# Masks added by TensorE for the first five attention units, in a fused attention and mixture-of-experts kernel

## The chip, the cores and the metric

The kernel runs on one core of a Trainium2 chip. The metric is the device time of one execution in microseconds, median of several runs. An engine is named by what it does here: TensorE multiplies (matmul and transpose) into PSUM, VectorE (DVE) and ScalarE (ACT) read PSUM and SBUF, GpSimd (POOL) works on SBUF alone, SyncE (SP) issues most DMAs.

## The reference, cut to what matters

Three layers, one after the other: masked attention, a dense layer pair, and a sparse expert layer with skipping. The change touches only the attention of batch 0.

```python
# q, k, v: (4, 8, 576, 64)
rel = pos[:, None] - pos[None, :]
mask_local   = (rel >= 0) & (rel < 32)                         # heads 0..3
mask_strided = (rel >= 0) & (pos[None] % 32 == pos[:, None] % 32)  # heads 4..7
scores = where(mask, q @ k.T / sqrt(64), -1e9)
attn = exp(scores - max(scores)); attn /= sum(attn) + 1e-9
x = attn @ v                                       # 2304 x 512
h = x @ w_in                                       # 512 -> 2048
g = where(h >= 1, h, where(h <= -1, 0, (h + 1)**2 / 4))
x = g @ w_out                                      # 2048 -> 512
# then: rows with x @ w_skip <= 0 stay; the others go through one of 8 experts
```

## The kernel before, in words

**Units.** Attention is cut into units: one batch, one pair of heads (a "pair", one head in each half of the 128 partitions), and a few query tiles. Pairs 0 and 1 are local: a tile is 96 queries by 128 keys, so a unit of four tiles has scores of 96 x 512 for each head of the pair. Pairs 2 and 3 are strided: queries and keys are sorted by position modulo 32 on the host, a tile is 72 x 72, a unit is 72 x 288 for each head. Units 0 and 1 are local, 2 to 5 strided; all six belong to batch 0 and stand ahead of the main loop. The two heads are called halves below (`hh` 0 and 1).

**Jobs.** Each engine has a written order of jobs for the six units ahead of the loop (the strings `PE_BEFORE`, `DVE_BEFORE`, `ACT_BEFORE`, `POOL_BEFORE`), executed strictly in that order. The letters:

- S, TensorE (L845): score products of a unit, 16 matmuls in 64-row tiles, into two banks of PSUM.
- M, VectorE (L1177, L1181): for each half one scalar_tensor_tensor reads the bank, multiplies by 1/8, adds the mask and writes `prob_first` in SBUF; then for each half a negated maximum of every row of every tile, into `row_max`. The bank is free after the first of these.
- D, GpSimd (L1735): for unit 5 only, adds the negated maximum to the scores.
- X, ScalarE (L1577): exponentials in `prob_first`, one instruction for each tile, with the negated maximum as bias; for unit 5 (L1572) one for each half.
- K, GpSimd (L1745, L1748): partial sums of the rows of units 0 and 1. E, VectorE: the sums and their reciprocals.
- G, GpSimd (L1755): scales the exponentials by the reciprocals.
- P, TensorE (L861): transposes; C, ScalarE (L1590): copies them out of the bank. V, TensorE (L881): times the values. H, ScalarE (L1598) and L, VectorE (L1219): the result x as a rounded part and a rest.
- W, ScalarE (L1637) and R, GpSimd (L1785): the first `w_in` tiles as a rounded part and a rest.

**Banks.** PSUM has eight banks; `bank_table()` gives them to S (two), P (two) and V (one) jobs in rotation. A job waits until the use before it on its bank has been read out (`take_bank`).

**Fillers.** `FILLERS` says how many products of 128x512 bfloat16 on the tile `warm` (L825) stand ahead of a job. They compute nothing; "Q" is the second half of a P job. The list starts after eight more such products.

**Loop.** 96 steps follow (six chunks of 384 tokens, 16 feature tiles each): TensorE does `hidden` (L1042, twelve products) and `output` (L1058) and between them the jobs of later attention units, at places of `places_of_chunk`. The first step needs the results of all six units (`x_hi_ready`, `x_ready`) and the first weight remainder R0. Unit 6 and 7 are the rest of the local pairs of batch 0. Unit 8 (S at place 7 of chunk 0, after step 3's first half) is the first of batch 1 and waits for its own load of q and k, which SyncE issues after all weights.

**Loads.** SyncE issues loads in one written order (the first q and k, the identity, more q and k with the strided mask between them, v, three tiles of `w_in`, one of `w_out`, the rest of q, k, v, then the remaining weights alternately, then batch 1). ScalarE issues two: the first keys, and the local mask (L1681). VectorE waits for the local mask before its first job.

The code that the diff touches:

## Time and profile before

| | us |
|---|---|
| median of 3 runs | 503.79 (503.68 to 503.83) |
| the profiled execution | 503.48 |
| its span | 501.7 |
| TensorE busy | 493.4 (98%) |
| TensorE weight loads | 426.3 (85%) |
| VectorE busy | 251.8 (50%) |
| ScalarE busy | 192.9 (38%) |
| GpSimd busy | 218.1 (43%) |

The span is the stretch between the first and the last instruction of the profiled execution; the execution's own time is 1.8 us longer. Busy shares are means over the whole span. The stage ahead of the loop lasts about 26.6 us and has quite other shares than the rest, so it has to be read by windows. Instructions of one engine overlap a little at their ends, so that the distance from start to start is shorter than the duration that the rows show. The ends of matmuls are modelled. "issue" in a chain is time in which the engine waited for nothing that the profile shows, and "DVEq" is the instruction queue of VectorE.

### The profile page before, as it was taken

The page shows a single profiled execution, that of the slowest core. Times are in us where ns is not written, and L with a number is a line of the kernel's source. Part 1 is how long each engine was busy: PE and PEld are TensorE (multiplying, and loading weights), DVE is VectorE, ACT ScalarE, POOL GpSimd, SP SyncE. Part 2 cuts the span into 40 slices and gives each one's busy share as a digit, 9 for nine tenths or more (in the row PEclk, how much of TensorE's full clock was granted, in tenths as well). Part 3 has the DMA queues.
Part 4 walks back from the last instruction along what each step waited for, and adds up shares of the span by engine and source line. Part 5 has one row for each costly group of instructions (what it writes and reads, how often), then busy time and mean ns, then how long its engine had stood idle before and what let it go on. Part 6 is the DMA issues. An engine that isn't in the chain of part 4 may idle for free.

```text
span 501.7 us, 8901 instructions
## 1 busy us (share of the span) xinstructions
PE 493.4 (98%) x3429; PEld 426.3 (85%) x3429; DVE 251.8 (50%) x593; ACT 192.9 (38%) x429; POOL 218.1 (43%) x245
## 2 busy tenths in 40 slices
PE   8999999999999999999999999999999999999996
PEld 4688888889988888888888888888998898888895
DVE  5876657634335536666525666652445342332322
ACT  4956456543223324353423343442322222222222
POOL 2978966852223324465423555642222312222221
PEclk9999999999999999999999999999999999999999
DMA  8993220103001204202110421000300017850001
GB/s 282 354 386 110 73 78 5 52 2 127 0 7 42 74 25 174 80 2 82 49 48 15 160 82 33 1 2 18 125 2 1 1 40 297 294 169 1 2 0 67
DMA packets 18977, 42.15 MB, mean 84 GB/s; under 512 B 2054, under 2 KB 3920, under 8 KB 18932
## 3 DMA queue, kind: packets, MB, share of 16 engines
q1 hardware_dynamic: 18580, 41.13, 23.9%
q8 instruction: 28, 0.46, 0.4%
q10 hardware_dynamic: 256, 0.41, 0.3%
q14 instruction: 17, 0.14, 0.1%
q0 software_dynamic: 96, 0.02, 0.0%
HBM read 32.94 MB, written 8.78 MB: 83 GB/s over the span
## 4 chain that ended last, share of the span: by engine, by line
PE 93%; DVE 3%; ACT 2%; POOL 1%; issue 1%; DVEq 0%
PE bank L1058 39%; PE bank L1042 39%; PE bank L881 4%; PE bank L845 4%; PE bank L861 3%; PE bank L825 1%; PE bank L985 1%; PE bank L966 1%; POOL part_sums L1745 1%; DVE prob L1193 1%; ACT g_hi L1704 0%; DVE bank L1186 0%; DVE row_max L1191 0%; POOL part_sums L1748 0%; ACT prob L1580 0%
## 5 line engine op out<-in xcount | busy, mean ns | idle before, releaser
L1824 POOL TENSOR_TENSOR g_lo<-act_f,g_hi 128x384 fp32r<-128x384 f32 x96 | 97.3, 1014 | 197.1 <-ACT g_hi L1704 196.6
L1695 ACT ACTIVATE act_f<-act_f,half_col 128x384 f32<-128x384 f32 x96 | 59.1, 615 | 201.0 <-DVE act_f L1431 200.9
L1431 DVE TENSOR_SCALAR act_f<-bank 128x384 f32<-128x384 f32 x96 | 53.3, 555 | 146.5 <-PE bank L1042 141.5
L1042 PE MATMUL bank<-x_hi,win_hi 128*128 128x384 f32 x384 | 87.7, 347 | 0.6 <-DVE act_f L1434 0.6
L1058 PE MATMUL bank<-wout_hi,g_hi 128*128 128x512 f32 x285 | 85.0, 406 | 0.0
L1704 ACT CAST g_hi<-act_f 128x384 fp32r<-128x384 f32 x96 | 49.1, 512 | 92.0 <-DVE act_f L1434 91.7
L1042 PE MATMUL bank<-x_hi,win_lo 128*128 128x384 f32 x384 | 83.9, 337 | 0.0
L1042 PE MATMUL bank<-x_lo,win_hi 128*128 128x384 f32 x384 | 83.2, 335 | 0.0
L1058 PE MATMUL bank<-wout_lo,g_hi 128*128 128x512 f32 x285 | 81.1, 393 | 0.0
L1058 PE MATMUL bank<-wout_hi,g_lo 128*128 128x512 f32 x285 | 81.0, 392 | 0.0
L1042 PEld LDWEIGHTS bank<-x_hi,win_hi 128*128 128x128 f32 x384 | 66.7, 188 | 8.3 <-issue 1.5
L1434 DVE TENSOR_TENSOR act_f<-act_f,bank 128x384 f32<-128x384 f32 x96 | 52.5, 547 | 36.7 <-ACT act_f L1695 33.1
L1042 PEld LDWEIGHTS bank<-x_hi,win_lo 128*128 128x128 f32 x384 | 69.6, 188 | 0.0
L1042 PEld LDWEIGHTS bank<-x_lo,win_hi 128*128 128x128 f32 x384 | 68.1, 188 | 0.2 <-DVEq L1222 0.2
L1058 PEld LDWEIGHTS bank<-wout_lo,g_hi 128*128 128x128 f32 x285 | 53.5, 188 | 12.6
L1058 PEld LDWEIGHTS bank<-wout_hi,g_lo 128*128 128x128 f32 x285 | 53.5, 188 | 12.3
L1058 PEld LDWEIGHTS bank<-wout_hi,g_hi 128*128 128x128 f32 x285 | 49.9, 188 | 6.8 <-issue 0.6
L1755 POOL TENSOR_TENSOR prob<-prob,row_sum 72x288 f32<-72x288 f32 (+2 forms) x52 | 37.8, 746 | 23.5 <-DVE row_sum L1214 23.5
L1735 POOL TENSOR_TENSOR prob<-prob,row_max 72x288 f32<-72x288 f32 (+1 forms) x32 | 25.7, 821 | 28.0 <-DVE row_max L1181 28.0
L1219 DVE TENSOR_TENSOR x_lo<-bank,x_hi 128x288 fp32r<-128x288 f32 (+2 forms) x32 | 18.8, 586 | 30.3 <-ACT x_hi L1598 29.7
L1208 DVE TENSOR_REDUCE sum_terms<-prob 72x4 f32<-72x288 f32 (+2 forms) x52 | 23.2, 487 | 5.0 <-ACT prob L1580 5.0
L1790 POOL TENSOR_TENSOR wout_lo<-wout_raw,wout_hi 128x512 fp32r<-128x512 f32 x16 | 20.5, 1284 | 10.8 <-ACT wout_hi L1641 10.8
(135 smaller groups left out, 423.4 us busy)
## 6 DMA issues: line engine op xcount, KB each, us to landing
w_early<-in_w_dram SPq DMA_DIRECT2D x4, 2048.0 KB, 9.0
qk<-in_qk_dram SPq DMA_DIRECT2D x12, 592.0 KB, 4.9
out_dram<-y_rows SPq DMA_DIRECT2D x18, 256.0 KB, 2.6
win_raw<-in_w_in_dram SPq DMA_DIRECT2D x16, 256.0 KB, 9.3
wout_raw<-in_w_out_dram SPq DMA_DIRECT2D x16, 256.0 KB, 9.6
y_dram<-y_rows SPq DMA_DIRECT2D x15, 256.0 KB, 3.0
v<-in_v_dram SPq DMA_DIRECT2D x6, 384.0 KB
v<-in_v_dram SPq DMA_DIRECT2D x6, 288.0 KB
```

The source lines that it names most:

```text
L845: mm = pe.matmul(bank_of("S", n, hh)[0:rows, width * i:width * (i + 1)], buf[head, q_at:q_at + rows], buf[head, k_at:k_at + width], start= ...
L1042: mm = pe.matmul(h_ps[s % 2][:, 0:CH], w[:, f, P * k:P * (k + 1)], x[:, k, cols], start=(at == 0), stop=(at == len(order) - 1))
L1058: mm = pe.matmul(y_ps[t][:, :], g[:, s % RING, P * t:P * (t + 1)], w[:, f, :], start=(f == 0 and i == 0), stop=(f == FT - 1 and i == 2))
L1208: dve.tensor_reduce(sum_terms[0:unit_rows(u), hh, 0:u.nt, 0], tiled(u, hh), AX.X, ALU.add)\
L1431: dve.tensor_scalar(tile, h_ps[s % 2][:, 0:CH], -1.0, 1.0, ALU.max, ALU.min).then_inc(clip_ready, 1)
L1434: dve.tensor_tensor(tile, tile, h_ps[s % 2][:, 0:CH], ALU.max).then_inc(act_ready, 1)
L1695: act.activation(tile, tile, ACT.Square, bias=half_col[:, 0:1], scale=0.5).then_inc(square_ready, 1)
L1704: act.copy(g_hi[:, s % RING, :], tile).then_inc(g_hi_ready, 1)
L1735: pool.tensor_tensor(tiled(u, hh), tiled(u, hh), over_tiles(u, peak_of(u, hh)), ALU.add)\
L1755: pool.tensor_tensor(tiled(u, hh), tiled(u, hh), over_tiles(u, sums_of(u, hh)), ALU.mult)\
L1790: pool.tensor_tensor(wout_lo[:, f, :], wout_raw[:, f, :], wout_hi[:, f, :].bitcast(F32), ALU.subtract)\
L1824: pool.tensor_tensor(g_lo[:, s % RING, :], act_f[:, s % 2, :], g_hi[:, s % RING, :].bitcast(F32), ALU.subtract).then_inc(g_lo_ready, 1)
```

## The change

For units 0 to 4 (`PE_MASKS = 5`) the mask is no longer added by VectorE:

- TensorE's S job ends with one more product for each half: the identity (in bfloat16) times the mask tile (in bfloat16, 0 or -2^33), accumulated onto the scores in the bank. 2^33 is large enough that the later factor 1/8 leaves it below -1e9.
- VectorE's M job becomes, for each half, a negated maximum straight from the bank (96x512 or 72x288), a wait for it, and a multiplication of these maxima by 1/8 (96x4 or 72x4).
- ScalarE's X job reads the bank instead of `prob_first`, with scale 1/8 and the scaled maximum as bias, and writes `prob_first`. The bank is free only when the exponentials of its half are done: the semaphore `exp_ready` stands in for `bank_free`.
- Three constants are added to the constant table (local mask, identity, strided mask as bfloat16 pairs in float32 words). ScalarE's second DMA loads them as one tile `mask_words` of 96 x 448 words in place of the float32 local mask (96 x 512 words). SyncE loads the float32 local mask later, after the first `w_out` tile (unit 6 waits for it), and the float32 strided mask after the q and k of pairs 2 and 3.
- The four orders and the fillers are new. Fillers ahead of the loop, beyond the first eight: 34 before, 30 after. V0 stands before P1, P3 before V1, V3 before P5; VectorE has E3 before M5 and L0 before E5; ScalarE swaps W0 and H0, and C4 and H3; GpSimd has G3 before D5.

```diff
--- before.py
+++ after.py
@@ -36,6 +36,7 @@
 TILES_UP = -(-SLOTS // SPAN) * SPAN
 FAR = float(1 << 17)
 MASKED = -1e9
+FAR_BELOW = -float(1 << 33)
 SCRATCH = 4096
 
 CH = 384
@@ -88,6 +89,7 @@
 UNITS = all_units()
 N_PRO = 6
 SHIFTED = 5
+PE_MASKS = 5
 POOL_SUMS = 2
 REST = 2
 PER_BATCH = 8
@@ -112,13 +114,13 @@
 
 
 
-PE_BEFORE = "S0 S1 S2 S3 S4 P0 S5 P1 V0 P2 V1 P3 V2 V3 P4 P5 V4 V5"
-DVE_BEFORE = "M0 M1 M2 E0 M3 E1 M4 E2 M5 E3 E4 E5 L0 L1 L2 L3 L4 L5"
-ACT_BEFORE = "X0 X1 X2 X3 C0 X4 W0 C1 C2 H0 X5 C3 H1 H2 H3 C4 C5 H4 H5 W1 W2"
-POOL_BEFORE = "K0 K1 G0 G1 G2 D5 G3 G4 G5 R0 R1 R2"
-
-
-FILLERS = {("S", 1): 2, ("S", 2): 6, ("P", 0): 14, ("Q", 0): 2, ("P", 1): 2, ("Q", 1): 1, ("P", 2): 1, ("V", 1): 2, ("P", 3): 1, ("P", 5): 1, ("V", 4): 2}
+PE_BEFORE = "S0 S1 S2 S3 S4 P0 S5 V0 P1 P2 P3 V1 V2 P4 V3 P5 V4 V5"
+DVE_BEFORE = "M0 M1 M2 E0 M3 E1 M4 E2 E3 M5 E4 L0 E5 L1 L2 L3 L4 L5"
+ACT_BEFORE = "X0 X1 X2 X3 C0 X4 H0 C1 C2 W0 X5 C3 H1 H2 C4 H3 C5 H4 H5 W1 W2"
+POOL_BEFORE = "K0 K1 G0 G1 G2 G3 D5 G4 G5 R0 R1 R2"
+
+
+FILLERS = {("S", 1): 2, ("S", 2): 6, ("P", 0): 12, ("Q", 0): 2, ("V", 0): 1, ("P", 1): 1, ("Q", 1): 2, ("P", 2): 1, ("V", 1): 1, ("P", 5): 1, ("V", 4): 1}
 
 
 def jobs_of(names):
@@ -213,6 +215,13 @@
 
 BANKS, PRO_USES = bank_table()
 
+READ_BY_EXP = {BANKS["S", n][hh]: (n, hh) for n in range(PE_MASKS) for hh in range(2)}
+
+
+def frees(bank, use):
+
+    return use - sum(b == bank and k <= use for b, k in READ_BY_EXP)
+
 
 def constants():
     r = np.arange(P)
@@ -223,11 +232,17 @@
     strided_mask = (res[:, None] == res[None, :]) & (pos[:, None] >= pos[None, :])
     fill = lambda keep: np.where(keep, 0.0, MASKED)
     token = r[:, None] + P * np.arange(NT)[None, :]
+    as_bf16 = lambda a: (np.ascontiguousarray(a, dtype=np.float32).view(np.uint32) >> 16).astype(np.uint16)
+    in_words = lambda a: as_bf16(a).view(np.float32)
+    far = lambda keep: np.where(keep, 0.0, FAR_BELOW)
     parts = {
         "ident": np.eye(P),
         "mask_local": np.concatenate([fill(first)] + [fill(local)] * 3, axis=1),
         "mask_strided": np.concatenate([fill(strided_mask)] * 4, axis=1),
         "add_groups": (r[:, None] % GROUP == np.arange(E + 1)[None, :]) * 1.0,
+        "local_words": in_words(np.concatenate([far(first)] + [far(local)] * 3, axis=1)),
+        "ident_words": in_words(np.eye(TQ)),
+        "strided_words": in_words(np.concatenate([far(strided_mask)] * 4, axis=1)),
         "from_here": (r[:, None] >= r[None, :]) * 1.0,
         "ones": np.ones((P, P)),
         "expert_order": np.tile(np.arange(E, 0, -1)[None, :], (P, 1)),
@@ -330,6 +345,18 @@
         assert at <= steps_end
         prob_t_first = [sb(f"prob_t_first{i}", [P, 2, 4 * TQ], F32, offset=prob_at + 4 * 2 * 4 * TQ * i)
                         for i in range(2)]
+
+
+        words_from = columns["local_words"][0]
+        words = {n: (columns[n][0] - words_from, columns[n][1], columns[n][2])
+                 for n in ("local_words", "ident_words", "strided_words")}
+        n_words = sum(width for _, _, width in words.values())
+        assert n_words <= S
+        mask_words = sb("mask_words", [TQ, n_words], F32, offset=x_at + 4 * S)
+
+        def in_bf16(name):
+            at, rows, width = words[name]
+            return mask_words[0:rows, at:at + width].bitcast(BF16)
 
         mask_l = sb("mask_l", [TQ, 4 * TK], F32)
         mask_s = sb("mask_s", [TS, 4 * TS], F32)
...
@@ -536,17 +564,21 @@
 
         def wait_free(eng, kind, n, i=0):
             bank, use = BANKS[kind, n][i]
-            eng.wait_ge(bank_free[bank], use)
+            eng.wait_ge(bank_free[bank], frees(bank, use))
 
         def take_bank(eng, kind, n, i=0):
             bank, use = BANKS[kind, n][i]
-            if use > 1:
-                eng.wait_ge(bank_free[bank], use - 1)
+            if (bank, use - 1) in READ_BY_EXP:
+                unit, hh = READ_BY_EXP[bank, use - 1]
+                eng.wait_ge(exp_ready, 2 * unit + hh + 1)
+            elif use > 1:
+                eng.wait_ge(bank_free[bank], frees(bank, use - 1))
 
         def wait_pro_banks(eng, which):
             for bank in which:
                 if PRO_USES[bank] > 0:
-                    eng.wait_ge(bank_free[bank], PRO_USES[bank])
+                    assert (bank, PRO_USES[bank]) not in READ_BY_EXP
+                    eng.wait_ge(bank_free[bank], frees(bank, PRO_USES[bank]))
 
 
         def qk_of(u):
@@ -692,9 +724,9 @@
             sp.dma_start(qk_main[0][:, 0:4 * TQ], qk[0, 0, :, 0:4 * TQ]).then_inc(qk_loaded[0], 16)
             constant(ident, "ident", ident_loaded)
             first_tiles(1)
-            constant(mask_s, "mask_strided", mask_s_loaded)
             load_qk(0, 2)
             load_qk(0, 3)
+            constant(mask_s, "mask_strided", mask_s_loaded)
             for p in range(2):
                 sp.dma_start(v_main[p][:, 0:4 * P], v[0, p, :, 0:4 * P]).then_inc(v_loaded[p], 16)
             load_v(0, 2)
@@ -702,6 +734,7 @@
             for f in range(3):
                 load_w_in(f)
             load_w_out(0)
+            constant(mask_l, "mask_local", mask_l_loaded)
             rest_tiles(0)
             rest_tiles(1)
             sp.dma_start(w_score[:, :, :], w_score_dram[:, :, :]).then_inc(scores_loaded, 16)
@@ -844,9 +877,16 @@
                         head = slice(D * hh, D * hh + D)
                         mm = pe.matmul(bank_of("S", n, hh)[0:rows, width * i:width * (i + 1)],
                                        buf[head, q_at:q_at + rows], buf[head, k_at:k_at + width],
-                                       start=True, stop=True)
-                        if i == u.nt - 1:
+                                       start=i == 0 or n >= PE_MASKS, stop=n >= PE_MASKS)
+                        if i == u.nt - 1 and n >= PE_MASKS:
                             mm.then_inc(full_sem("S", n, hh), 1)
+                if n < PE_MASKS:
+                    if n == 0:
+                        pe.wait_ge(mask_words_loaded, 16)
+                    for hh in range(2):
+                        pe.matmul(bank_of("S", n, hh)[0:rows, 0:u.nt * width], in_bf16("ident_words")[0:rows, 0:rows],
+                                  in_bf16("strided_words" if strided(u.p) else "local_words"), start=False,
+                                  stop=True).then_inc(full_sem("S", n, hh), 1)
 
             def transpose_probs(n):
                 u = UNITS[n]
@@ -1161,10 +1201,21 @@
             def masked_scores(n):
                 u = UNITS[n]
                 cols = u.nt * unit_width(u)
+                if n < PE_MASKS:
+                    for hh in range(2):
+                        wait_full(dve, "S", n, hh)
+                        by_tile = scores_of(u, hh).rearrange("p (i w) -> p i w", w=unit_width(u))
+                        dve.tensor_reduce(peak_of(u, hh), by_tile, AX.X, ALU.max, negate=True).then_inc(peaks_ready, 1)
+                        dve.wait_ge(peaks_ready, 2 * n + hh + 1)
+                        dve.tensor_scalar(peak_of(u, hh), peak_of(u, hh), D ** -0.5, None, ALU.mult)\
+                           .then_inc(max_ready, 1)
+                    return
                 if strided(u.p):
                     dve.wait_ge(mask_s_loaded, 16)
                     mask = mask_s[:, :]
                 else:
+                    if n == N_PRO:
+                        dve.wait_ge(mask_l_loaded, 16)
                     mask = mask_l[:, 0:cols] if u.t0 == 0 else mask_l[:, TK:TK + cols]
                 if N_PRO <= n < N_PRO + 2:
                     wait_full(dve, "V", n - N_PRO)
@@ -1415,7 +1466,6 @@
             dve.memset(half_col[:, :], 0.5).then_inc(half_ready, 1)
             dve.memset(sum_terms[:, :, :, :], 1e-9).then_inc(terms_ready, 1)
             dve.wait_ge(terms_ready, 1)
-            dve.wait_ge(mask_l_loaded, 16)
             for kind, n in jobs_of(DVE_BEFORE):
                 if kind == "M":
                     masked_scores(n)
@@ -1572,9 +1622,11 @@
                         a = act.activation(prob_of(u, hh), prob_of(u, hh), ACT.Exp)
                     elif n < SHIFTED:
                         act.wait_ge(max_ready, 2 * n + hh + 1)
+                        width = unit_width(u)
                         for i in range(u.nt):
-                            tile = tiled(u, hh)[:, i, :]
-                            a = act.activation(tile, tile, ACT.Exp, bias=peak_of(u, hh)[:, i:i + 1])
+                            scored = bank_of("S", n, hh)[0:unit_rows(u), width * i:width * (i + 1)]
+                            a = act.activation(tiled(u, hh)[:, i, :], scored, ACT.Exp,
+                                               bias=peak_of(u, hh)[:, i:i + 1], scale=D ** -0.5)
                     else:
                         act.wait_ge(shift_ready, 2 * (n - N_PRO) + hh + 1)
                         a = act.activation(prob_of(u, hh), prob_of(u, hh), ACT.Exp)
@@ -1677,8 +1729,8 @@
 
             act.dma_start(qk_main[0][:, QC:QC + PAD + 4 * TQ], qk[0, 0, :, QC:QC + PAD + 4 * TQ])\
                .then_inc(qk_loaded[0], 16)
-            at, rows, width = columns["mask_local"]
-            act.dma_start(mask_l[:, :], table_dram[0:rows, at:at + width]).then_inc(mask_l_loaded, 16)
+            act.dma_start(mask_words[:, :], table_dram[0:TQ, words_from:words_from + n_words])\
+               .then_inc(mask_words_loaded, 16)
             for kind, n in jobs_of(ACT_BEFORE):
                 if kind == "X":
                     exponentials(n)
```

## Rows read from the trace of the kernel before

**Rows 1.** The page, part 4: the chain that ended last, by engine.

```profile
PE 93%; DVE 3%; ACT 2%; POOL 1%; issue 1%; DVEq 0%
```

**Rows 2.** Busy microseconds in two stretches: engines PE, PEld, DVE, ACT, POOL, clock, DMA.

```profile
10.00:15.00 5.00, 4.03 (x42) 2.05 (x39) 4.86 (x17) 5.00 (x20) 4.76 (x9) 1.00 1.03 292
26.50:43.00 16.50, 15.93 (x106) 13.56 (x104) 12.19 (x30) 11.36 (x26) 13.81 (x14) 1.00 0.87 325
```

**Rows 3.** The chain in order of time, 0 to 30 us: start, duration, what.

```profile
5.78 1.28 DVE prob_first L1177 x2
...
7.70 1.29 ACT prob_first L1577 x4
...
13.95 1.01 POOL prob_first L1755
...
16.55 0.67 PE bank L845 x16
...
18.64 0.81 PE bank L881 x16
...
26.61 2.41 PE bank L1042 x12
```

**Rows 4.** TensorE's timeline ahead of the loop: start, busy, instruction, count, idle before.

```profile
4.52 1.12 PE L845 MATMUL bank<-qk 64*96 64x128 f32 x16
...
6.67 1.12 PE L845 MATMUL bank<-qk 64*96 64x128 f32 x16 [0.49 <-DMA qk<-in_qk_dram]
...
7.72 1.47 PE L825 MATMUL bank<-warm 128*128 128x512 bf16 x6
...
9.12 1.78 PE L845 MATMUL bank<-qk_first 64*72 64x72 f32 x48
...
10.84 3.19 PE L825 MATMUL bank<-warm 128*128 128x512 bf16 x14
...
15.00 0.55 PE L861 MATMUL bank<-ident,prob_first 96*128 96x96 f32 x4 [0.97 <-POOL prob_first L1755]
...
16.00 0.55 PE L861 MATMUL bank<-ident,prob_first 96*128 96x96 f32 x4
...
24.86 0.60 PE L825 MATMUL bank<-warm 128*128 128x512 bf16 x2
```

**Rows 5.** ScalarE's timeline, the same columns.

```profile
7.70 8.75 ACT L1577 ACTIVATE prob_first<-prob_first,row_max 96x128 f32<-96x128 f32 x32 [4.77 <-DVE row_max L1181]
...
16.35 0.83 ACT L1590 COPY prob_t_first<-bank 128x384 f32<-128x384 f32 x2
...
17.08 2.07 ACT L1577 ACTIVATE prob_first<-prob_first,row_max 72x72 f32<-72x72 f32 x8
...
21.26 0.79 ACT L1572 ACTIVATE prob_first<-prob_first 72x288 f32<-72x288 f32 x2
```

**Rows 6.** GpSimd's timeline, the same columns.

```profile
20.40 3.96 POOL L1755 TENSOR_TENSOR prob_first<-prob_first,row_sum 72x288 f32<-72x288 f32 x6
...
24.32 1.28 POOL L1785 TENSOR_TENSOR win_lo<-win_raw,win_hi 128x512 fp32r<-128x512 f32 x1
```

**Rows 7.** Groups by line and shape: busy us, mean ns of one, idle before.

```profile
L1181 DVE TENSOR_REDUCE row_max<-prob_first 96x4 f32<-96x512 f32 x4 | 2.5, 672 | 0.0
...
L1371 DVE TENSOR_SCALAR left_flags<-score 128x3 bf16<-128x3 f32 x1 | 0.2, 170 | 0.0
...
L1590 ACT COPY prob_t<-bank 72x288 f32<-72x288 f32 x8 | 2.8, 403 | 0.1
```

**Rows 8.** Loads (KB, us to landing), SyncE's issue of batch 1, S8's first weights.

```profile
mask_l<-shape_constants ACTq DMA_DIRECT2D x1, 192.0 KB, 4.2
...
30.93 2.06 SPq L659 DMA_DIRECT2D qk<-in_qk_dram  x2
...
qk<-in_qk_dram SPq DMA_DIRECT2D x1, 592.0 KB, 10.5
...
42.73 0.60 PEld L845 LDWEIGHTS bank<-qk 64*72 64x72 f32 x16
```

More of the change, by code:

```diff
@@ L399, in build @@
         ids = [sb(f"ids{i}", [P, 1], U32) for i in range(2)]
-        r_table = sb("r_table", [P, sum(columns[n][2] for n in list(columns)[4:])], F32)
-        assert list(columns)[4] == "from_here"
+        r_table = sb("r_table", [P, sum(columns[n][2] for n in list(columns)[7:])], F32)
+        assert list(columns)[7] == "from_here"
         best = sb("best", [P, NT], F32)
@@ L445, in build @@
         ident_loaded = sem("ident_loaded")
+        mask_words_loaded, peaks_ready = sem("mask_words_loaded"), sem("peaks_ready")
         mask_l_loaded, mask_s_loaded = sem("mask_l_loaded"), sem("mask_s_loaded")
```

## The prediction

> **What bounds the kernel now.** I read the page first: nearly all of the chain that ended last is TensorE [rows 1], with the granted clock at 1.00 in every slice, so time is won only where TensorE waits or does work of no use. The windows by stage come next [rows 2]. From 26.5 us on TensorE is 97% busy and the loop over 96 steps pays for its own products. Before it, in the part that the change touches, ScalarE is full from 10 to 15 us (5.00 of 5.00), VectorE (4.86) and GpSimd (4.76) nearly, and TensorE's 4.03 is padded with filler products on the tile `warm`. The third view is the chain in order of time [rows 3]: score products of unit 0, VectorE's mask (L1177), row maxima, exponentials at 7.70, GpSimd's partial sums and scaling at 13.95, TensorE, and the loop's first product (L1042) at 26.61. So this change is worth what it moves that first product, as long as nothing with a fixed arrival stands behind it.
>
> **The start of the exponentials.** Before, the bank of unit 0 is full at 4.52 + 1.12 = 5.64, the masking pair begins at 5.78, the first exponential at 7.70 [rows 3, 4]. After, a mask product follows the scores. The pattern of the second unit gives its start: a full-width product begins 0.07 before the modelled end of the score products (6.67 + 1.12 = 7.79 against 7.72), so 5.57. It lasts 0.38 (a lone filler: 3.19 less 13 pitches of 0.216), and the bank is full at 5.95. Then 0.04 for a semaphore (GpSimd ends at 13.95 + 1.01, TensorE starts at 15.00), the maximum over 512 columns at 0.67 [rows 7], 0.04, the new scaling of the 96x4 maxima, 0.04. That small op is not in the trace: the nearest row is a TENSOR_SCALAR of 128x3 at 0.17 [rows 7]; its bounds are 0 (wholly overlapped) and 0.4 (two of them, if the wait ahead of it costs as much again). With 0.17 the exponentials start at 6.91, that is 0.79 earlier. The mask words are no larger than the mask they replace (96 rows of 1792 bytes for 2048) and leave from the same place; that one landed 4.2 us after its issue at 1.16, at 5.31 to 5.36 [rows 8], before the 5.57 where they are wanted. VectorE gains too: a local unit costs 2 x (0.67 + 0.04 + about 0.1) = 1.6, where the masking alone took 1.28 and as many maxima stood behind it [rows 3]. It was full but late for nobody except through these jobs; I book nothing more.
>
> **GpSimd.** It starts on the first exponentials' end, so its run K0, K1, G0 also moves 0.79: unit 0's scaled probabilities are ready at 14.20 where TensorE took them at 15.00 after 0.97 us of idling [rows 4].
>
> **TensorE's front, which takes the gain back.** Added are two mask products per unit, one per half. Unit 1: 2 x 0.216 = 0.43. Units 2 to 4: 288 columns at that rate, 0.12 each, 0.24 a unit, 0.72. Each also turns the array from pairs of 64-row tiles to full height and back. From rows: sixteen 72-wide products and one turn take 0.67 (at 16.55 [rows 3]); forty-eight and one turn take 9.12 to 10.84, 1.72; so sixteen cost 0.525 and the turn 0.145. The way back costs 0.10 (six fillers end at 7.72 + 1.30 = 9.02, S2 starts at 9.12). Two more round trips: 0.48. Sum 1.63: the fillers before P0 start at 12.46, not 10.83. There are twelve now (2.59 us), so P0 can start at 15.05, as late as before, with its data waiting since 14.20. The wait for the first of these banks (now until X1's exponentials end, about 11.6) is over by 12.46; S4, which now waits for X0, finds it done at about 9.3. The Trainium skill, "TensorEngine Tiling (Array Packing)", section Tiling Modes, says that changing the tiling mode drains TensorE; the 0.145 and 0.10 above agree, and without such turns the sum would give P0 at 14.57.
>
> P0's second half waited for GpSimd until 16.00; now it follows at 15.05 + 0.33 + two fillers (0.43) = 15.81. That 0.19 and what ScalarE had too much is the gain here: ScalarE was busy with exponentials up to 16.35, and copied P0 after them, in 2 x 0.37; X4 began at 17.08 [rows 5]. After, X0 to X3 end at 6.91 + 8.65 = 15.56; P0's second half is done at 15.81 + 0.55 (as long as its row at 16.00), its copy begins at 16.40 and takes 0.37, X4 comes at 16.77: 0.31 earlier.
>
> **ScalarE's exponentials from the bank.** No row shows an exponential with a bias that reads PSUM. From rows: a copy of 72x288 out of a bank lasts 0.40 with the next 0.29 behind it [rows 7], the exponential of 72x288 in SBUF 0.45, the pair 0.79 [rows 5], so 0.34 apart. Bounds: 0.05 shorter each, or as much longer, because a second operand is applied. I take 0.04 shorter, and it is worth nothing in the sum: before P0 ScalarE already waits, and after X4 the copies of P1 wait for TensorE (P0's copy ends at 16.40 + 0.47; a filler 0.22, V0 0.81 [rows 3], a filler 0.22, half of P1 0.33, two fillers 0.43, the other half 0.55 and 0.04: its copy can begin at 19.5. ScalarE wants it at 16.77 + 1.98 for X4, 0.37 for H0, 0.37 for the first half: 19.49). The Trainium skill, "VectorE: DVE Perf Modes", section on the TRN2 errata, gives ScalarE 224 cycles fixed from SBUF and 172 from PSUM; 52 cycles are an estimated 0.043 us, which the copy's row agrees with. By that page alone, 40 exponentials would save 1.7 us; by the chain above nothing.
>
> **The other orders.** Between X4 and X5 ScalarE does the same jobs in both orders (one W, C1, C2, one H), so X5 moves with X4: 20.95 for 21.26. GpSimd now does G3 before the shift D5; its own chain, six scalings to 24.36 before [rows 6], could end at 23.57, but the last two wait for unit 5's sums, which come 0.31 earlier: 24.05. P5's second half was held by TensorE's own queue: the fillers behind it start at 24.86 [rows 4]. With V3 pulled ahead it goes at 24.10, and the queue is free for the next at 24.35 (four transposes of 72 columns; for 96 columns four take 0.33, so I count 0.25): -0.51. One filler less before V4: -0.22. V4, V5 and the first product of the loop: -0.73, at 25.88. GpSimd's first weight remainder (R0, 1.28 from 24.32 [rows 6]) ends at 25.3, before it. Steps 0 to 2 are relative to that start (VectorE's work on unit 6, W1, R1), since unit 5's values H5, L5 move with V5.
>
> **DMA.** Strided mask and local mask move behind, but all are still loaded: the stream carries 168 KB more before the weights of the loop end. It is full until 40 us (0.87 busy from 26.5 to 43); at the 325 GB/s of that stage [rows 2] it is 0.5 us, at the rate of full DMA engines 325 / 0.87 = 374 it is 0.46. First to feel it is S8: its load, issued at 30.93, lands 10.5 later at 41.4 to 41.5, which becomes 41.9; TensorE wanted it at 42.73 [rows 8] and now wants it at 42.00. It just fits. The first w tile is wanted at 19 to 20 us and is sent ahead of the added bytes.
>
> **Sum.** 0.73 off the profiled execution's 503.48 gives 502.75; the median of the runs shown lies 0.31 above that execution, so 503.79 - 0.73 = 503.1.
>
> **Rivals.**
> (a) The front is not held by fillers: turns cheaper or hidden, P0 goes when its data is there. For: the idle of 0.97 before P0 shows there was room; GpSimd's own run allows 0.79 and three exponentials shortened by 0.04 another 0.12. Then the last scaling and P5 move 0.9, and with the filler saved it is 1.1: 502.7. Against: the count above.
> (b) The load of S8 or another fixed arrival takes part back, or the small scaling and its wait cost 0.2 a half on a full VectorE: gain 0.3, 503.5.
> (c) Slower: exponentials from a bank are dearer than from SBUF, and a bank is held until they are done. X0 to X3 end 0.84 before the copy of P0's second half, less the first half's copy of 0.37: that covers 0.47 / 32 = 0.015 us each. Beyond it every exponential counts up to X4; at 0.03 each the whole gain is gone, at 0.05 it is 40 x 0.05 - 0.47 - 0.73 = 0.8 slower, 504.6. Against: every bank-reading row of ScalarE is shorter than its SBUF sister.
> (d) Four fillers fewer (42 to 38) and mask products in bfloat16 let the granted clock fall from 2.4 to 1.2 GHz between 10 and 26 us. Products of some 5 us on the path would take twice that: 508. Against: TensorE's longest idle stretch shrinks, since P0's 0.97 goes.
>
> **Chances.** Forecast 0.47, (a) 0.25, (b) 0.15, (c) 0.08, (d) 0.05. One per 500 (0.2%, 1.0 us) is about what a measurement tells from none: faster by more is (a) and a tail, 0.27; slower is half of (c) and (d), 0.10; within it 0.63. The range 502.4 to 504.3 holds (a), (b) and most of (c); the forecast's own is 502.8 to 503.4.
>
> **What the new profile would show.** First exponential near 6.9; no idle of TensorE before P0, which starts near 15.0 behind its fillers (an idle there speaks for (a)); spacing of the 96x128 exponentials 0.25 where it was 0.29 (above 0.31 speaks for (c)); X5 near 20.9; the loop's first product near 25.8; S8 near 42.0; granted clock 1.00 throughout. A first product later than 26.3 makes the prediction wrong, as does a new idle above 0.5 us in the loop.

## The result, and the profile after

The changed kernel took 504.92 us in the median of ten executions (504.20 to 506.39), the kernel before 503.91 (503.37 to 504.48, ten) beside it: a ratio of 1.0020, 95% interval 1.0012 to 1.0028. It is slower by about 1.0 us. The forecast was 503.1, the range 502.4 to 504.3: the time is outside it.

The profiled execution took 504.68 (before 503.48), its span is 502.9 (before 501.7). The whole difference is there when the loop's step 0 is over: the last product of that step starts at 29.79 where it started at 28.58, and the last hidden product of the whole loop at 492.17 where it was 490.93. The loop itself is unchanged, so only the first 30 us need to be read.

TensorE's timeline of the changed kernel (start, busy, instruction, count, idle before), to be laid beside [rows 4]:

```profile
4.57 1.43 PE L878 MATMUL bank<-qk 64*96 64x128 f32 x16
5.92 0.63 PE L887 MATMUL bank<-mask_words 96*96 96x512 bf16 x2
...
6.92 1.12 PE L878 MATMUL bank<-qk 64*96 64x128 f32 x16
...
9.82 0.74 PE L878 MATMUL bank<-qk_first 64*72 64x72 f32 x16
10.50 0.44 PE L887 MATMUL bank<-mask_words 72*72 72x288 bf16 x2
...
12.85 2.75 PE L858 MATMUL bank<-warm 128*128 128x512 bf16 x12
15.44 0.49 PE L901 MATMUL bank<-ident,prob_first 96*128 96x96 f32 x4
...
25.16 0.91 PE L901 MATMUL bank<-ident,prob_first 72*72 72x72 f32 x8
...
27.37 0.80 PE L1082 MATMUL bank<-x_hi,win_hi 128*128 128x384 f32 x3
...
29.79 0.45 PE L1082 MATMUL bank<-x_lo,win_hi 128*128 128x384 f32 x1 [0.23 <-DVEq L1273]
```

TensorE no longer waits before P0: the idle of 0.97 us is gone, and its fillers fill the time, as forecast. But the loop's first product stands at 27.37, not at the forecast 25.88, and 0.83 later than before. ScalarE and GpSimd, the same columns (for [rows 5] and [rows 6]):

```profile
7.38 8.10 ACT L1628 ACTIVATE prob_first<-bank,row_max 96x128 f32<-96x128 f32 x32 [4.46 <-DVE row_max L1210]
...
17.11 1.77 ACT L1628 ACTIVATE prob_first<-bank,row_max 72x72 f32<-72x72 f32 x8
...
21.92 0.44 ACT L1622 ACTIVATE prob_first<-prob_first 72x288 f32<-72x288 f32 x1 [0.28 <-POOL prob_first L1787]
```

```profile
13.43 4.04 POOL L1807 TENSOR_TENSOR prob_first<-prob_first,row_sum 96x512 f32<-96x512 f32 x4
18.73 2.54 POOL L1807 TENSOR_TENSOR prob_first<-prob_first,row_sum 72x288 f32<-72x288 f32 x4 [1.25 <-DVE row_sum L1265]
...
24.23 1.29 POOL L1807 TENSOR_TENSOR prob_first<-prob_first,row_sum 72x288 f32<-72x288 f32 x2 [0.47 <-DVE row_sum L1265]
```

GpSimd used to run through from 13.95; now it stands still for 1.25 us at 17.48, waiting for the reciprocal of unit 2's sums on VectorE. So VectorE is what to read. There the maxima now read the bank and the masking is gone; the new kind of job is the scaling (L1210):

```profile
13.98 0.53 DVE L1210 TENSOR_SCALAR row_max<-row_max 72x4 f32<-72x4 f32 x1
...
15.62 0.89 DVE L1210 TENSOR_SCALAR row_max<-row_max 72x4 f32<-72x4 f32 x1
16.42 0.44 DVE L1208 TENSOR_REDUCE row_max<-bank 72x4 f32<-72x288 f32 x1
16.90 0.60 DVE L1210 TENSOR_SCALAR row_max<-row_max 72x4 f32<-72x4 f32 x1
17.42 0.80 DVE L1259 TENSOR_REDUCE sum_terms<-prob_first 72x4 f32<-72x288 f32 x2
...
18.45 0.20 DVE L1265 RECIPROCAL row_sum<-row_sum 72x8 f32<-72x8 f32 x1
```

A scaling of 72x4 values takes between 0.17 and 0.89 us. The long ones have something in common that these rows show when they are laid against GpSimd's: its four scalings of unit 0 and 1 run from 13.43 in steps of 1.01, so they change over at 14.44, 15.45, 16.46 and end at 17.47, and VectorE's end at 13.98 + 0.53 = 14.51, 15.62 + 0.89 = 16.51 and 16.90 + 0.60 = 17.50. Taken one by one, those three GpSimd instructions end at 14.48, 16.48 and 17.48, so each long scaling ends 0.02 to 0.03 after the instruction that was running when it began, as if it had waited for it. The two other long ones (9.96 + 0.59 and 11.34 + 0.41) end as close behind a partial sum of GpSimd's. The two at 7.18 and 7.97, before GpSimd's first, take 0.17. Three more (0.19 at 9.14, 0.17 at 12.14 and at 13.42) began 0.05 to 0.16 before the end of GpSimd's running instruction and had next to nothing to wait for. The ten together take 3.89 us (0.17, 0.17, 0.19, 0.59, 0.41, 0.17, 0.17, 0.53, 0.89, 0.60) where ten of 0.17 are 1.7.

A second loss shows on VectorE at the end of the units:

```profile
27.68 0.72 DVE L1270 TENSOR_TENSOR x_lo<-bank,x_hi 128x288 fp32r<-128x288 f32 x1 [1.27 <-ACT x_hi L1650]
28.98 0.70 DVE L1270 TENSOR_TENSOR x_lo<-bank,x_hi 128x288 fp32r<-128x288 f32 x1 [0.57 <-DVE x_lo L1270]
```

L4 and L5 (the low parts of unit 4's and 5's rows) are 1.30 us apart, where they were 0.87 apart before, with 0.57 us between them in which no data was missing. TensorE's last product of step 0 waits for L5: that step takes 2.42 us from first to last product instead of 2.04. So +0.83 up to the first product and +0.38 in step 0 make the 1.21.

One part of the +0.83 need not come from the change. The granted clock rose from 1.2 to 2.4 GHz at 4.23 in the profiled execution of before and at 5.24 in this one, so unit 0's scores took 1.43 where they took 1.12, and P0 came at 15.44; in two of the variants below, with the same work ahead of it and the rise at 4.31 and 4.45, P0 is at 15.03 and 15.10. In the profiled executions of all thirteen kernels of this document the rise lies between 3.87 and 7.06: 5.1 in the mean of the nine with masks on TensorE, 5.0 in the mean of the four without. To compare two profiles without this scatter, the distance from P0 to the loop's first product serves: 27.37 - 15.44 = 11.93 here.

### The profile page after: what moved, and what is told of

It reads as the page before. It is cut to its first block, busy times and chain, and to the rows that moved or that the text cites. A ratio compares the mean times of both kernels' runs of the same rounds, so it can differ in the third digit from the quotient of the medians.

```text
span 502.9 us, 8912 instructions
## 1 busy us (share of the span) xinstructions
PE 495.5 (99%) x3435; PEld 428.0 (85%) x3435; DVE 251.1 (50%) x593; ACT 192.5 (38%) x429; POOL 218.2 (43%) x245
## 4 chain that ended last, share of the span: by engine, by line
PE 92%; DVE 4%; ACT 2%; issue 1%; POOL 1%; DVEq 0%
PE bank L1098 39%; PE bank L1082 38%; PE bank L878 4%; PE bank L921 4%; PE bank L901 3%; PE bank L858 1%; PE bank L1025 1%; PE bank L1006 1%; DVE row_max L1210 1%; DVE prob L1244 1%; POOL prob_first L1807 1%; ACT g_hi L1756 0%; DVE bank L1237 0%; DVE row_max L1208 0%; DVE row_max L1242 0%
```

## The experiments

Theory P: a scaling from SBUF to SBUF stretches to the end of GpSimd's running instruction. Theory F: the gap between L4 and L5 is a property of the place in VectorE's instruction list. Rivals: the new orders are to blame, or the mask products with the longer front that they make. The edits below are to the changed kernel unless another is named.

**One operand from the bank.** The same sizes, the same waits, the same result of the small op; only its kind and the place of a second operand that it ignores differ.

```diff
-dve.tensor_scalar(peak_of(u, hh), peak_of(u, hh), D ** -0.5, None, ALU.mult)
+dve.scalar_tensor_tensor(out=peak_of(u, hh), in0=peak_of(u, hh), scalar=D ** -0.5,
+                         in1=bank_of("S", n, hh)[0:unit_rows(u), 0:u.nt], op0=ALU.mult, op1=ALU.bypass)
```

> The changed kernel, with the ten small scalings of the maxima given a second operand in PSUM that is passed over (scalar_tensor_tensor, bypass), so that VectorE reads one operand from SBUF at the width of one stream; values, waits and orders are the same. Theory P (the small TENSOR_SCALAR waits for the instruction that GpSimd is running, because both need the same way into SBUF; five of ten lasted 0.41 to 0.89 us and ended with GpSimd's instruction): all ten last 0.2 or less, VectorE wins back about 2.2 us by 17.5, GpSimd's gap of 1.25 before unit 2's scaling goes, the loop's first product comes 0.8 to 1.1 earlier than 27.37 (about 26.4), time about 504.0. Theory O (the new orders lose it) and theory M (the mask products on TensorE and the exponentials that hold the banks lose it): as the changed kernel, 504.9 within 0.2, first product at 27.3.

Measured: 504.13 (503.30 to 504.49), ratio to before 0.9997 (0.9988 to 1.0006). The profile of this kernel for that line (count, duration in ns as least/median/most), and the same line of the changed kernel:

```profile
L1210 DVE SCALAR_TENSOR_TENSOR row_max<-row_max,bank x10: 153/154/155, 7.3 to 15.6; 72x4 f32<-72x4 f32 x6, 96x4 f32<-96x4 f32 x4
```

```profile
L1210 DVE TENSOR_SCALAR row_max<-row_max x10: 165/300/885, 7.2 to 16.9; 72x4 f32<-72x4 f32 x6, 96x4 f32<-96x4 f32 x4
```

And its GpSimd timeline:

```profile
13.49 6.54 POOL L1808 TENSOR_TENSOR prob_first<-prob_first,row_sum 96x512 f32<-96x512 f32 x8
19.98 1.29 POOL L1788 TENSOR_TENSOR prob_first<-prob_first,row_max 72x288 f32<-72x288 f32 x2
```

TensorE's P0 and the loop's first product:

```profile
15.51 0.49 PE L901 MATMUL bank<-ident,prob_first 96*128 96x96 f32 x4
...
26.56 0.79 PE L1082 MATMUL bank<-x_hi,win_hi 128*128 128x384 f32 x3
```

All ten take 0.154, GpSimd runs without the gap before unit 2's scalings, and the loop's first product comes at 26.56, 0.81 before the changed kernel's, with the clock's rise at 5.39 against 5.24. From P0 it is 11.05 us instead of 11.93. This is the larger part of the loss, shown. The edit changes two things at once, the kind of instruction and the place of an operand; which of them takes the stretch away it does not say.

**No scaling at all** (the maxima go unscaled into the exponentials, so the shift is another one).

```diff
-dve.tensor_reduce(..., negate=True).then_inc(peaks_ready, 1)
+dve.tensor_reduce(..., negate=True).then_inc(max_ready, 1)
-dve.wait_ge(peaks_ready, 2 * n + hh + 1)
-dve.tensor_scalar(peak_of(u, hh), peak_of(u, hh), D ** -0.5, None, ALU.mult).then_inc(max_ready, 1)
```

> The changed kernel without the ten scalings: the exponentials take the unscaled maxima as bias, so each row is shifted by another constant; the part left out is the multiplication of the maxima by 1/8 and the wait ahead of it. Theory P: VectorE saves 2.2 us of stretched operations and ten times 0.2 of their own; first product 26.2 to 26.5, time 503.7 to 504.0, and no more than 0.3 below the run with the PSUM operand. Theories O and M: 504.7 to 504.9, since an engine with spare time is relieved.

Measured: 503.92 (503.16 to 505.92), ratio 0.9997 (0.9987 to 1.0008): no better than the ten short scalings. The gap of GpSimd is gone. In its profiled execution the q/k tiles of unit 1 came late (S1 at 8.00, TensorE idle for 1.33 before it), so its first product, 27.57, cannot be compared as it stands. From P0 (16.52) it is 11.05, the same as with the ten short scalings, so these cost nothing. L4 and L5 are 0.87 apart in it.

**The new orders alone**, on the kernel before: PE_BEFORE, DVE_BEFORE, ACT_BEFORE, POOL_BEFORE and FILLERS from the changed kernel, nothing else.

> The kernel before with the four orders and the fillers of the changed one; masks stay on VectorE. Theory O: slower than before by 0.7 or more. Theories P and M: between 0.3 faster and 0.3 slower than before; by my own count of the queues 0.15 faster (the loop's first product at 26.4 for 26.54).

Measured: 503.81 (503.32 to 505.36), ratio 0.9998 (0.9988 to 1.0007). The orders cost nothing and bring nothing by themselves that these runs can tell; the 0.15 expected is below what they resolve.

**The masks in the old orders**, the reverse: the changed kernel with those five lists from before.

> The changed kernel with the four orders and the fillers of the kernel before. Theory P: the small operations are stretched here too (some 2 us in sum), the loop's first product comes after 27.0, time 504.6 to 505.5. Theory O: equal to the kernel before or faster, 503.3 to 503.9. Theory M: slower than before as well, but with small operations of 0.2 and GpSimd never waiting for VectorE's sums.

Measured: 505.31 (503.98 to 506.68), ratio 1.0023 (1.0013 to 1.0034), as slow as the change. The scalings are stretched again (six of 72x4 with a mean of 0.46 us), GpSimd waits:

```profile
POOL prob_first L1807 <- DVE row_sum L1265: 1.3, 1, 1.3
```

(engine, line, waited for: us in total, times, longest). So the loss comes with the masks and not with the orders. It is not the scalings alone here: L4 and L5 are 1.30 apart in this kernel too, and its fourteen fillers keep P0 8.95 behind S1 (16.71 - 7.76) where twelve make it 8.52, 0.43 more. That the scaling is what the masks bring along rests on the two runs before this pair.

**Ten small scalings in the kernel before**, after each row maximum of units 0 to 4, on tiles that nothing else reads or writes. A memset at the start fills the source tile, so there are eleven VectorE instructions more.

```diff
 dve.tensor_reduce(peak_of(u, hh), tiled(u, hh), AX.X, ALU.max, negate=True).then_inc(max_ready, 1)
+if n < SHIFTED:
+    dve.tensor_scalar(extra_out[0:unit_rows(u), 2 * n + hh, 0:u.nt],
+                      extra[0:unit_rows(u), hh, 0:u.nt], D ** -0.5, None, ALU.mult)
```

> The kernel before, masks on VectorE, with a TENSOR_SCALAR of 96x4 or 72x4 in SBUF behind each of the ten row maxima of units 0 to 4; its result is used by nobody and nobody waits for it. Theory P (it waits for GpSimd's running instruction): four or more of the ten last over 0.3, ending within 0.1 of the end of a GpSimd instruction, 1.5 to 2.5 us of VectorE lost in sum; VectorE was full there, so the loop's first product comes 0.8 to 2 later than before. Against it: all ten last 0.2, and the run is as the one with memsets.

**The same with ten memsets** of the same output in their place; the first memset stays.

> The same places, but a MEMSET of 96x4 or 72x4 in place of each TENSOR_SCALAR: it writes SBUF and reads nothing. Theory P: all ten last 0.2 or less, together 0.6 to 1.2 us of VectorE, and the time is 0.7 or more below the run with the TENSOR_SCALARs, 0 to 0.8 above the kernel before. Against it: the two runs are equal.

Measured: 509.06 (508.51 to 509.57), ratio 1.0100 (1.0084 to 1.0115), and 507.02 (506.94 to 507.59), ratio 1.0058 (1.0045 to 1.0072). The groups of VectorE by shape, up to 20 us, of the one and of the other (busy us, mean ns | idle before):

```profile
L1186 DVE TENSOR_SCALAR extra_out<-extra 72x4 f32<-72x4 f32 x6 | 2.6, 437 | 0.0
...
L1186 DVE TENSOR_SCALAR extra_out<-extra 96x4 f32<-96x4 f32 x4 | 0.7, 180 | 0.0
```

```profile
L1186 DVE MEMSET extra_out<- 72x4 f32 x6 | 0.4, 62 | 0.0
```

The 2.0 us between the two are the stretched scalings, in a kernel that has nothing else of the change: from P0 to the loop's first product it is 13.66 us with the scalings (15.35 to 29.01) and 11.54 with the memsets (15.75 to 27.29), as in before (15.00 to 26.54). The mechanism does not need the mask products. But the expectation for the memsets was 0 to 0.8 us above before, and they cost 2.9. Those are not in the front, by the same 11.54. They are at the end. The memset kernel's span ends 5.2 us after its last VectorE operation (505.4; 500.06 + 0.15), that of before 2.6 after (501.7; 498.95 + 0.15). By the trace's records of branches and drains, VectorE's last branch is at 501.73 and its next instruction at 505.08, 3.35 us later; in before they are at 500.26 and 500.87, 0.61 apart, in the scaling kernel 503.52 and 506.39, 2.87. The DMA queues show one fetch of instructions alone after all others, at 505.7, that is 0.6 after that late instruction and not ahead of it. The memset kernel from 502.8 to 507.5 (DMA busy tenths in 40 slices, then the queue):

```profile
DMA  0000000000000000000000002000000000000000
...
q14 instruction: 1, 0.01, 0.6%
```

In before no fetch starts later than 501.5. Eleven instructions more made VectorE's exit longer, in both of these kernels; that its instructions were not at hand there is a guess, and the lone fetch does not show it, since it comes after. In the changed kernel, which has no more VectorE instructions than before, the branch takes 0.61 (501.50 to 502.11): this is a cost of the experiment, not of the change. The two kernels have it alike to 0.5 us (3.35 and 2.87), so their difference stands.

**Theory F: the list shifted by three.** In VectorE's list L5 is the 66th recorded instruction (waits that left a record counted) in before and in the orders alone, the 53rd without the scalings, the 77th in the two kernels with the extra small operations, and all five have 0.87 us ahead of it; it is the 63rd in the three kernels that have 1.30. Three memsets ahead of the list move it on (it is the 65th recorded then, one wait having left no record), here on the kernel with the operand from the bank:

```diff
+for i in range(3):
+    dve.memset(pad_out[:, i, :], 0.0)
 for kind, n in jobs_of(DVE_BEFORE):
```

> The run with the PSUM operand, with three memsets more at the start of VectorE's list, where it idles. In the three kernels whose last x rest (L5) is VectorE's 63rd recorded instruction, L5 starts 1.30 after L4, in the others (66th, 53rd) 0.87. Theory F (VectorE's instruction stream is refilled at a fixed place, and there it falls between L4 and L5): with three more the spacing goes back to 0.87, the loop's first step (first to last product) takes 2.04 and not 2.42, 0.4 less time: 503.7 where the run with the PSUM operand had 504.1. Against it: spacing 1.30 and 504.1.

Measured: 503.78 (503.39 to 504.12), ratio 0.9994 (0.9985 to 1.0003). In its profile L4 and L5 are 0.88 apart and step 0 takes 2.06; the medians alone could not show this 0.4, for the ratio without the memsets was 0.9997 and the two intervals overlap. And later the same three on the changed kernel as it is:

> The changed kernel with three memsets ahead of VectorE's list and nothing else. Theory F (the 1.30 us between L4 and L5, where before has 0.87, is the point at which VectorE's instructions are refilled): L4 to L5 goes back to 0.87 to 0.88 us, the loop's step 0 from 2.42 to 2.05 us, while the small scalings stay stretched (sum of ten near 4 us) and G2 stays near 18.7: median 0.4 us below the changed kernel's, 504.5. Rival (the gap comes from VectorE's late exit from the units, so from the scalings): L4 to L5 stays at 1.30 and the median at 504.9.

Measured: 504.46 (503.86 to 505.17), ratio 1.0006 (0.9997 to 1.0015). VectorE and GpSimd of this last one:

```profile
27.28 1.61 DVE L1271 TENSOR_TENSOR x_lo<-bank,x_hi 128x288 fp32r<-128x288 f32 x2 [1.27 <-ACT x_hi L1653]
```

```profile
18.31 2.53 POOL L1810 TENSOR_TENSOR prob_first<-prob_first,row_sum 72x288 f32<-72x288 f32 x4 [1.25 <-DVE row_sum L1266]
```

L4 and L5 run as one group again, 0.88 apart, step 0 takes 2.04, and GpSimd's wait of 1.25 is untouched: the two losses are separate, and the gap goes with what stands ahead in the list. That it is a refill of the instructions is an inference; no record names it.

**Fewer fillers.** With both losses gone the bound is the queue of twelve fillers at P0, as forecast: this takes four of them out of the kernel with the operand from the bank and the three memsets.

```diff
-FILLERS = {... ("P", 0): 12, ...}
+FILLERS = {... ("P", 0): 8, ...}
```

> As the run with pads, with eight fillers ahead of P0 instead of twelve. My prediction's account of TensorE's front: with twelve, P0 starts behind its fillers 0.9 after its data is ready (15.51 against 14.56 in the run with the PSUM operand); with eight it starts about 0.86 earlier, X5 0.5 to 0.8 earlier, the loop's first product 0.4 to 0.6 earlier, time 503.1 to 503.4. Against it (the fillers hold nothing, or the granted clock falls without them): equal, or slower with a clock below 0.99.

Measured: 503.45 (502.40 to 506.43), ratio 0.9991 (0.9974 to 1.0008), in two groups: eight executions from 502.40 to 504.13 and three at 506.11, 506.33 and 506.43. The profiled one is of the second group. Its TensorE timeline, and its windows by stage (PE, PEld, DVE, ACT, POOL, then granted clock, DMA share, GB/s):

```profile
41.69 0.55 PE L922 MATMUL bank<-prob_t,v 128*64 128x96 f32 x8
44.77 1.22 PE L879 MATMUL bank<-qk 64*72 64x72 f32 x16 [2.54 <-DMA qk<-in_qk_dram]
```

```profile
44.00:46.00 2.00, 1.23 (x17) 1.13 (x17) 0.00 (x0) 0.00 (x0) 2.00 (x2) 0.71 0.39 110
46.00:48.00 2.00, 2.00 (x6) 2.00 (x7) 1.91 (x5) 0.00 (x0) 1.34 (x2) 0.50 0.04 15
48.00:50.00 2.00, 2.00 (x11) 1.86 (x11) 1.11 (x3) 0.03 (x1) 0.00 (x0) 0.94 0.00 0
```

The loop had begun at 25.95, and unit 8's scores then waited 2.54 us for their q/k tiles; when that idle stretch ended, at 44.8, the granted clock went from 2.4 to 1.2 GHz, until 48.2. The kernel with the twelve fillers and the memsets had already waited there for 0.54:

```profile
43.30 0.74 PE L879 MATMUL bank<-qk 64*72 64x72 f32 x16 [0.54 <-DMA qk<-in_qk_dram]
```

So a transfer had become the next bound. SyncE issues it at the end of the stream of weights, at 32.77 there (33.87 with eight fillers) against 30.93 before [rows 8].

**That load ahead of the last four weight loads**, with twelve and with eight fillers (its buffer is free once unit 6's scores are done; no weight is late by it; at its old place, behind unit 6's scores in SyncE's later list, the load is left out, which the cut below does not show):

```diff
 for f in range(3, FT):
+    if f == FT - 1:
+        wait_full(sp, "S", N_PRO, 0)
+        wait_full(sp, "S", N_PRO, 1)
+        load_qk(1, 2)
     load_w_in(f)
     load_w_out(f - 2)
```

> The kernel with the bank as the scaling's second operand and the three memsets, and the q/k load of unit 8 issued ahead of SyncE's last four weight loads instead of behind them. Theory D (unit 8's scores wait for this load, which stands at the end of the stream of weights): the wait of 0.54 us ahead of S8 goes. Since the wait of 0.51 us before V8 at 50.3 us of the kernel before had gone with that one, it comes back, and the median stays: 503.8 us. Rival (the wait at S8 is the time itself): median 0.5 lower, 503.3.

> The same with 8 fillers at P0 instead of 12. Theory D: the loop's first product at 25.9 to 26.1 us as with 8 fillers before, S8 without the 2.54 us wait, the granted clock at full speed from its rise to the end in every execution, so no execution near 506; median 0.5 below before: 503.3 to 503.5. Rival C (the clock falls because of the fewer fillers, not because of the wait at S8): some executions stay at 506. Rival N (what the front gains is given back at the next late transfer or at V8): 503.8.

Measured, twelve fillers: 503.84 (502.96 to 504.33), ratio 0.9992 (0.9983 to 1.0001). Eight fillers: 502.87 (502.45 to 503.50, nine executions), ratio 0.9976 (0.9966 to 0.9986). With twelve the wait at unit 8 is gone and another is back that the late load had covered, as expected:

```profile
42.29 0.74 PE L883 MATMUL bank<-qk 64*72 64x72 f32 x16
...
50.37 0.55 PE L926 MATMUL bank<-prob_t,v 128*64 128x96 f32 x8 [0.51 <-ACT prob_t L1650]
```

(before has this second wait too, 0.51 at the same job; the kernel without the early load has none there). With eight, none of nine executions is near 506, where three of eleven were. That speaks against the fillers as the cause of the falling clock; nine are few, and the 2.54 us wait is the better evidence, from one profiled execution. The 502.87 is below the 503.3 to 503.5 that was expected. This kernel is faster than before by 1.2 us (0.24% of 504), and by the ratios than the changed kernel too; its own profiled execution is the slowest of the nine, with unit 1's tiles late (S1 at 7.70), and is not used for sizes.

## Why the prediction was wrong

**The step that failed** is the small scaling on VectorE. The prediction priced it at 0.17, bounded it by 0 and 0.4, and said of VectorE's list that it "was full but late for nobody except through these jobs; I book nothing more". The 0.17 came from a TENSOR_SCALAR at 498 us [rows 7], where GpSimd does nothing. Beside GpSimd's instructions the same kind of op takes up to 0.89, outside the upper bound, and 0.39 in the mean of the ten, hardly inside it. The rest of the ten it counted at about 0.1 each, with their waits, and booked nothing for what they do to a full VectorE. The 2.2 us that the ten cost in excess made E2 late, GpSimd stood for 1.25 us before unit 2's scalings, and everything behind them moved: ScalarE's X5 came at 21.92 for 20.95, TensorE's P5 at 25.16. Rival (b) had this place ("the small scaling and its wait cost 0.2 a half on a full VectorE") but gave it 0.4 us of a lost gain; it was 0.81, and more than the gain. The range needed that rival on the far side of zero.

What would have shown it: GpSimd 4.76 busy of 5 us in [rows 2], and the rule for just this pair. The Trainium skill, "SBUF — State Buffer", section Who interferes with whom, says that VectorE and GpSimd share one pair of SBUF ports, that a VectorE operation in a two-port mode (a tensor_scalar can enter one) and a GpSimd instruction exclude each other for a whole instruction, and that an operation with at most one SBUF input outside these modes does not contend. The trace agrees: the stretched scalings end 0.02 to 0.03 us after GpSimd's instruction, and as a SCALAR_TENSOR_TENSOR with one operand in PSUM all ten take 0.154. By that rule a scaling beside a 1.01 us instruction should have been priced at up to 1 us.

**The second loss** (0.38 in step 0) was in no step and no rival. It hangs on where L5 falls in VectorE's list. No row of before shows it.

**The sum against the forecast.** The loop's first product was 1.49 later than forecast (27.37 for 25.88). Of this 0.39 are there at P0 (15.44 for 15.05), and go with the clock's later rise in this execution. 0.88 arise between P0 and the first product, by the scalings (11.93 for 11.05). The last 0.22 is missing in the kernels without the stretch as well (11.05 for the forecast 10.83).

**What held.** The first exponential: forecast 6.91, measured 6.88 and 6.96 in the executions of the variants whose granted clock rose at 4.31 and 4.45 us; in the changed kernel, with the rise at 5.24, the first exponential came at 7.38. The forecast had taken over the early rise of before's profiled execution without saying so. Where the rise came as late as it often does, the forecast is off by 0.47, so that the two early executions hit it is in part luck. TensorE's front: from S1 to the end of the mask products 5.79 us forecast, 12.85 - 6.92 = 5.93 measured. The mask products and turns: a strided unit with its mask 10.86 - 9.82 = 1.04, forecast 0.525 + 0.145 + 0.24 + 0.10 = 1.01. No idle before P0, so rival (a) is out. The exponentials from the bank are shorter, not longer, by just the 0.04 taken: the eight of unit 4, which run without a wait, take 1.77 for 2.07 [rows 5], 0.30 over seven distances, and from start to start it is 0.250 us for 0.292 at 96x128 and 0.203 for 0.245 at 72x72. The run of 32 hides this (8.10 for 8.75), because ScalarE waits for a scaled maximum at four places in it. The prediction's estimated 0.043 is borne out. Rival (c) is out, and (d) for this kernel, whose clock stays up once risen.

**The size of the gain without the losses.** The kernel with twelve fillers and the early load has P0 at 15.03 (forecast 15.05) and the loop's first product at 26.08, against 26.54 before: -0.46, where -0.73 was forecast.

```profile
15.03 0.49 PE L906 MATMUL bank<-ident,prob_first 96*128 96x96 f32 x4
...
26.08 0.80 PE L1087 MATMUL bank<-x_hi,win_hi 128*128 128x384 f32 x3
```

From P0 to the first product it takes 11.05, the forecast 10.83. Nearly all of these 0.22 are there at X5, which stands 6.10 behind P0 (21.13) where 5.90 was forecast: ScalarE waits 0.29 for the second half of C1 (at 19.55, 4.52 behind P0, forecast 4.45), and behind that wait it now does W0 (0.52 to the next start) in the place of H0 (0.37). The prediction counted the same jobs in both orders and did not ask on which side of the wait they stand. P5's second half then waits 0.25 for GpSimd. The gain of 0.46 reaches the end (last hidden product 490.49 for 490.93), and the median is 0.39 lower (503.84 for 504.23), with an interval that just touches no change.

**S8's load "just fits"** did not hold either, once tested. The added 168 KB were counted at 0.46 us; in the kernel with the memsets the load was issued 1.84 later than before and its tiles were there at 43.30, not at 41.9. This did no harm in the changed kernel only because everything else was late as well (S8 at 43.94, no wait). A part of the rest is lost early: from 10 to 15 us the stream moves 292 GB/s before [rows 2], 274 in the changed kernel and 265 in the one with the memsets, and from 15 to 20 us 352, 328 and 301, each time with the DMA engines full. For the kernel with the memsets these 27 and 51 GB/s are 0.39 MB in 10 us, an estimated 1.0 us at the 385 GB/s that it moves later. Why the stream is slower there stays open.

## What to carry to other kernels

Before adding a small SBUF-to-SBUF operation on VectorE, look at what GpSimd is doing in that stretch, and price the operation at the length of GpSimd's running instruction, not at its duration elsewhere in the trace; here a form of it with its second operand in PSUM was not stretched. Count every such operation on a full engine, also where only the first of them is on the path. Removing fillers or work from a front is worth only what the next fixed arrival allows: move that load first. And take the place of instructions as a cost of its own: three VectorE instructions more moved 0.4 us here, eleven moved 2.9. And before two profiles are compared from their start, look at when the granted clock rose in each.

## What the runs showed of the hardware

- A TENSOR_SCALAR of 96x4 or 72x4 float32 from SBUF to SBUF takes 0.17 us with GpSimd idle, and beside its TENSOR_TENSORs up to 0.89: it ends 0.02 to 0.03 us after the running one where that had more than 0.17 to go (five of ten in the changed kernel). A SCALAR_TENSOR_TENSOR with its second operand in PSUM takes 0.154, a MEMSET 0.06, beside the same GpSimd work.
- Two neighbouring VectorE instructions with all data ready start 0.87 or 1.30 us apart, by how many instructions stand ahead of them in the list (0.87 at the 53rd, 65th, 66th and 77th, 1.30 at the 63rd recorded).
- An exponential with a bias column, read from PSUM instead of SBUF, follows the one before it 0.042 us sooner (0.250 for 0.292 at 96x128, 0.203 for 0.245 at 72x72).
- With eleven more instructions in its program VectorE took 2.9 to 3.4 us from its last branch to the next instruction, where it takes 0.6 without them.
- After 2.54 us in which TensorE had nothing to do, the granted clock stood at 0.50 for about 3.4 us; after a wait of 0.54 us at the same place it did not fall. The first rise came between 3.87 and 7.06 us in thirteen profiled executions.
